# A gated recurrence and a squared-ReLU MLP on one core: other order of the first loads, three opening pairs by halves, second weights rounded one group ahead, a reordered last group

## What is computed

```python
# x, f_logit: (2, 6080, 256); lower_bound: (256,)
f = lower_bound + (1 - lower_bound) * sigmoid(f_logit)
h = f[:, t] * h + (1 - f[:, t]) * x[:, t]        # for t in range(6080), y[:, t] = h
# the MLP over all 12160 tokens; w_in: (256, 2048), w_out: (2048, 256)
hidden = y.reshape(12160, 256) @ w_in
g = maximum(hidden, 0) ** 2
out = g @ w_out
```

## Time and profile before

| | |
|---|---|
| median of 3 runs | 992.76 us (992.21 to 994.01) |
| the profiled execution | 992.73 us, of which its span is 990.7 us |
| PE busy | 985.3 us (99%), 4394 matmuls |
| PE weight loads busy | 819.2 us (83%) |
| DVE busy | 731.2 us (74%) |
| ACT busy | 697.3 us (70%) |
| POOL busy | 48.3 us (5%) |
| PE clock granted | full in all 40 slices |
| DMA | 8 tenths busy in the first slice (24.8 us), 309 GB/s; 42 GB/s over the span |
| the chain that ended last | PE 99%, DVE 1% |

### The profile page before, as it was taken

How to read it: one execution, slowest core, us unless ns; L and a number is a source line. 1 busy time by engine, 2 the same in 40 slices (tenths; PEclk the granted TensorE clock), 3 DMA queues, 4 the chain that set the end, 5 groups by cost and what they waited for, 6 DMA issues and landing times.

```text
span 990.7 us, 12612 instructions
## 1 busy us (share of the span) xinstructions
PE 985.3 (99%) x4394; PEld 819.2 (83%) x4394; DVE 731.2 (74%) x939; ACT 697.3 (70%) x924; POOL 48.3 (5%) x50
## 2 busy tenths in 40 slices
PE   9999999999999999999999999999999999999998
PEld 7898888888888888888888888888888888888887
DVE  6897876887787688687687768768768777876545
ACT  7876766776776776676677677677667767766665
POOL 2673000000000000000000000000000000000000
PEclk9999999999999999999999999999999999999999
DMA  8003011102101201100210110110111021001001
GB/s 309 21 1 109 14 43 43 43 1 85 43 1 43 85 0 42 64 21 0 85 42 0 55 72 0 42 64 21 34 51 42 0 85 43 1 0 43 1 1 43
DMA packets 22159, 41.95 MB, mean 42 GB/s; under 512 B 1521, under 2 KB 3313, under 8 KB 22129
## 3 DMA queue, kind: packets, MB, share of 16 engines
q1 hardware_dynamic: 21984, 41.43, 12.1%
q10 hardware_dynamic: 144, 0.13, 0.0%
HBM read 29.10 MB, written 12.45 MB: 42 GB/s over the span
## 4 chain that ended last, share of the span: by engine, by line
PE 99%; DVE 1%; issue 0%; ACT 0%; POOL 0%; DVEq 0%; ACTq 0%; POOLq 0%
PE out_ps L849 52%; PE hidden_ps L835 42%; PE hidden_ps L875 3%; PE out_ps L869 1%; PE out_ps L875 1%; PE out_ps L859 1%; DVE x_in L512 0%; DVE w_out_lo L613 0%; ACT g_hi L361 0%; POOL zeros L811 0%; DVE result L771 0%; DVE result L776 0%; DVE result L773 0%; DVE g_lo L625 0%; DVEq L775 0%
## 5 line engine op out<-in xcount | busy, mean ns | idle before, releaser
L849 PE MATMUL out_ps<-g_hi,w_out_hi 128*128 128x512 f32 (+1 forms) x760 | 294.3, 387 | 1.2 <-DVE w_out_lo L613 1.2
L849 PE MATMUL out_ps<-g_lo,w_out_hi 128*128 128x512 f32 (+1 forms) x760 | 294.1, 387 | 0.0
L849 PE MATMUL out_ps<-g_hi,w_out_lo 128*128 128x512 f32 (+1 forms) x760 | 294.1, 387 | 0.0
L625 DVE TENSOR_TENSOR g_lo<-h,g_hi 128x1024 fp32r<-128x1024 f32 (+1 forms) x190 | 232.6, 1224 | 69.8 <-ACT g_hi L361 66.8
L354 ACT ACTIVATE h<-h 128x1024 f32<-128x1024 f32 (+1 forms) x190 | 200.2, 1054 | 3.2
L849 PEld LDWEIGHTS out_ps<-g_hi,w_out_hi 128*128 128x128 f32 x760 | 142.6, 188 | 29.9 <-DVE w_out_lo L613 1.6
L849 PEld LDWEIGHTS out_ps<-g_lo,w_out_hi 128*128 128x128 f32 x760 | 142.7, 188 | 28.3
L849 PEld LDWEIGHTS out_ps<-g_hi,w_out_lo 128*128 128x128 f32 x760 | 142.6, 188 | 28.1
L835 PE MATMUL hidden_ps<-sums_hi,wc_hi 128*128 128x512 f32 x352 | 137.1, 389 | 0.0
L835 PE MATMUL hidden_ps<-sums_lo,wc_hi 128*128 128x512 f32 x352 | 137.0, 389 | 0.0
L835 PE MATMUL hidden_ps<-sums_hi,wc_lo 128*128 128x512 f32 x352 | 136.9, 389 | 0.0
(11 more groups left out here) (109 smaller groups left out, 1050.1 us busy)
## 6 DMA issues: line engine op xcount, KB each, us to landing
x_in<-x_t SPq DMA_DIRECT2D x22, 512.0 KB, 4.4
f_in<-f_logit_t SPq DMA_DIRECT2D x22, 512.0 KB, 4.7
out_t<-result SPq DMA_DIRECT2D x20, 512.0 KB, 3.1
w_in_raw<-w_in_t SPq DMA_DIRECT2D x8, 256.0 KB, 6.3
w_out_raw<-w_out_t SPq DMA_DIRECT2D x8, 256.0 KB, 7.3
x_in<-x_first SPq DMA_DIRECT2D x4, 224.0 KB, 5.4
out_t<-result SPq DMA_DIRECT2D x2, 448.0 KB, 3.0
out_t<-result SPq DMA_DIRECT2D x3, 256.0 KB, 2.0
```

Of the source, the lines that this page charges most:

```text
L625: nc.vector.tensor_tensor(g_lo[b][:, :, 0:n], h_of(it, j, b), g_hi[b][:, :, 0:n].bitcast(F32), ALU.subtract).then_inc(g_ready[b], 1)
L849: mm = nc.tensor.matmul(out_ps[:, b, c, 0:n], half[:, j, m, c * P:(c + 1) * P], moving[b][:, m, 0:n], start=(j == 0 and m == 0 and k == 0) ...
```

## The change

- The constants: 16 in place of 20 zero matmuls at the start, 2 in place of 4 between the halves.
- Loads: the second half's f is issued ahead of `w_in` 0, and `w_in` 2 ahead of batch 1's pieces.
- ACT: the second half's gate comes ahead of the rounding of `w_in` 0; `w_in` 2 is rounded right behind `w_in` 1, ahead of batch 1's gate and of `half_y_hi(1)`.
- DVE: `half_y_lo(0)` comes behind the second half's scans; `half_y_lo(1)` ahead of the rest of `w_in` 1.
- PE: three pairs of batch 0 instead of two are done by halves in their hi-by-hi pass; all passes with the lo values come in full width behind both halves.
- `w_out` 2 to 6 are each rounded, and their rests formed, one group earlier, `w_out` 1 earlier within the first group; `w_out` 7 stays where it is.
- The last group of the last tile has its own order, `last_quad`: the passes of the previous group's products are split among `product7`, `product4` and `product3`.

```diff
-WARM_UP = 20
-FILL = 4
+WARM_UP = 16
+FILL = 2
...
         def w_out_quads(j):
-            return (j, j + 1) if j == QUADS - 2 else (j,) if j < QUADS - 2 else ()
+            return (j + 1,) if j < QUADS - 1 else ()
...
             load_first_f(0, 0)
             load_first_x(0, 0)
+            load_first_f(0, 1)
             load_w_in(0)
-            load_first_f(0, 1)
             load_first_x(0, 1)
             load_w_in(1)
+            load_w_in(2)
             load_first_f(1, 0)
             load_first_x(1, 0)
             load_first_f(1, 1)
             load_first_x(1, 1)
-            load_w_in(2)
             load_w_out(0)
...
                 plain_w_in_hi(3)
                 first_relu(2, 0)
+                round_w_out(1)
                 first_relu(0, 1)
...
                 square_pair(0, 1, 1)
-                round_w_out(1)
+                round_w_out(2)
                 gate(1, 0, 0)
...
+            gate(0, 0, 1)
             plain_w_in_hi(0)
-            gate(0, 0, 1)
             for c in range(C):
                 half_forget(1, c)
             plain_w_in_hi(1)
+            plain_w_in_hi(2)
             gate(0, 1, 0)
             half_y_hi(1)
             first_forget(1, 0)
             gate(0, 1, 1)
             first_forget(1, 1)
-            plain_w_in_hi(2)
             first_y_hi(1, 0)
...
                     lo_pair(0, 0, 0)
+                    rest_of_w_out(1)
                     lo_pair(0, 0, 1)
                     lo_pair(0, 1, 0)
-                    rest_of_w_out(1)
+                    rest_of_w_out(2)
...
             first_w_in_lo(0)
-            half_y_lo(0)
             for c in range(C):
                 half_input(1, c)
                 half_scan(1, c)
+            for k in range(2):
+                half_y_lo(k)
             first_w_in_lo(1)
-            half_y_lo(1)
...
-            def first_two_pairs0():
+            def first_three_pairs0():
 
                 for k in range(2):
                     pe.wait_ge(first_hi_done[0][k], 1)
-                    for j in range(2):
+                    for j in range(3):
                         pe.wait_ge(w_plain_hi_done, j + 1)
                         for c in range(C):
 
                             first_part(j, 0, c, wc_hi, hi_of, opens=k == 0 and c == 0, columns=part(k))
-                        if j == 0:
+                        if (k, j) == (0, 0):
                             rests_of_w_in(0)
                             for c in range(C):
-                                first_part(0, 0, c, wc_lo, hi_of, columns=part(k))
-                        if k == 0:
-                            pe.wait_ge(first_ready[0][0], 1)
-                            for c in range(C):
-                                first_part(j, 0, c, wc_hi, lo_of, columns=part(0))
+                                first_part(0, 0, c, wc_lo, hi_of, columns=part(0))
                     if k == 0:
                         warm(FILL)
-                rests_of_w_in(1)
                 for c in range(C):
-                    first_part(1, 0, c, wc_lo, hi_of)
-                pe.wait_ge(first_ready[0][1], 1)
-                for j in range(2):
-                    first_part(j, 0, 0, wc_hi, lo_of, columns=part(1))
-                    first_part(j, 0, 1, wc_hi, lo_of, columns=part(1), signal=pair_done[0])
+                    first_part(0, 0, c, wc_lo, hi_of, columns=part(1))
+                for k in range(2):
+                    pe.wait_ge(first_ready[0][k], 1)
+                for j in range(3):
+                    first_part(j, 0, 0, wc_hi, lo_of)
+                    if j == 0:
+                        first_part(0, 0, 1, wc_hi, lo_of, signal=pair_done[0])
+                    else:
+                        first_part(j, 0, 1, wc_hi, lo_of)
+                        rests_of_w_in(j)
+                        first_part(j, 0, 0, wc_lo, hi_of)
+                        first_part(j, 0, 1, wc_lo, hi_of, signal=pair_done[0])
...
                 product5(it, odd, j)
+                if very_last(it, j):
+                    last_quad(it, odd, j, prev)
+                    return
...
+            def last_quad(it, odd, j, prev):
+
+                second(*prev, 0, 0, 1, passes=(0,))
+                product7(it, odd, j)
+                second(*prev, 0, 0, 1, passes=(1, 2))
+                second(*prev, 0, 1, 0, passes=(0, 1))
+                product4(it, odd, j)
+                second(*prev, 0, 1, 0, passes=(2,))
+                second(*prev, 0, 1, 1, passes=(0, 1))
+                product3(it, odd, j)
+                second(*prev, 0, 1, 1, passes=(2,))
+                second(*prev, 1, 0, 0)
```

More of the change, by code:

```diff
@@ L837, in product, with second @@
                 mm.then_inc(signal, 1)
-            def second(it, j, b, m, c):
+            def second(it, j, b, m, c, passes=range(3)):
                 n, q = width(it), it * QUADS + j
-                if m == 0 and c == 0:
+                if m == 0 and c == 0 and 0 in passes:
                     if narrow(it) and b == 0:
@@ L847, in second @@
                     pe.wait_ge(g_ready[b], q + 1)
-                for k, (half, moving) in enumerate(((w_out_hi, g_hi), (w_out_hi, g_lo), (w_out_lo, g_hi))):
+                for k in passes:
+                    half, moving = ((w_out_hi, g_hi), (w_out_hi, g_lo), (w_out_lo, g_hi))[k]
                     mm = nc.tensor.matmul(out_ps[:, b, c, 0:n], half[:, j, m, c * P:(c + 1) * P],
@@ L851, in second @@
                                           stop=False, skip_group_check=True)
-                if m == 1 and c == 1:
+                if m == 1 and c == 1 and 2 in passes:
                     mm.then_inc(g_used[b], 1)
@@ L965, in first_quad @@
                 if j == 0:
-                    first_two_pairs0()
-                    first_pair0(2)
+                    first_three_pairs0()
                     first_two_pairs1()
@@ L1032, in quad @@
                 second(*prev, 0, 1, 0)
-                if not very_last(it, j):
-                    second(*prev, 0, 1, 1)
+                second(*prev, 0, 1, 1)
                 product4(it, odd, j)
[L1036 to L1039, removed]
+                second(*prev, 1, 0, 0)
                 product3(it, odd, j)
-                if very_last(it, j):
-                    second(*prev, 1, 0, 0)
+                second(*prev, 1, 0, 1)
+                second(*prev, 1, 1, 0)
+                second(*prev, 1, 1, 1)
+            def last_quad(it, odd, j, prev):
[8 more added lines that the diff above has]
+                second(*prev, 0, 1, 1, passes=(2,))
+                second(*prev, 1, 0, 0)
                 second(*prev, 1, 0, 1)
```

## The result

The changed kernel takes 990.88 us (median of 22 runs, 990.22 to 991.84) against 992.70 (22 runs, 992.21 to 994.01): ratio 0.9982, 95% interval 0.9975 to 0.9988. That is 1.82 us less, where 1.62 was forecast, inside the range. The profiled execution is one of the slower ones: 991.41 us, span 989.4, so the two traces are only 1.32 apart. The other 0.5 us of the gain shows in the medians and not in these two executions.

The account below looks back on a forecast made before the run. TensorE (PE), busy 985.3 of 990.7 us, was taken as the bound. From the profiled 992.73, 0.24 + 0.03 lost and 1.48 + 0.41 gained gave -1.62, so 991.1; range 990.2 to 992.4, own range 990.6 to 991.6.

Parts of the forecast that it names:

- What bounds the kernel: Whole kernel: PE is busy for 985.3 of 990.7 us, so an edit counts only if it moves PE.
- The stall, 1.48: PE's wait for `w_out_lo` near 37 us goes when the second weights are rounded one group earlier: 1.48 us gained.
- What is late next: After the stall, `second(2,0)` and `second(3,0)`: VectorE is near full from 36 to 56 us, but no use comes nearer than 1.2 us.
- The last group, 0.41: Last group of the last tile: the new order puts the last products in place at 981.73, 0.41 us gained, bounds 0.15 to 0.5.
- DMA order: Opening loads: `w_in` 0 lands at 7.02 instead of 6.25, `w_in` 2 at 9.35, f of batch 1 at 10.06.
- Rivals A and B: Start: A, it gains a little, 990.7, chance 0.18; B, it loses more through late loads, 991.7, chance 0.15.
- Pairs' end, 17.25: Start: the three opening pairs on PE end at 17.25 instead of 17.01, 0.24 us lost.
- Warm-ups and fills worth nothing: Start: dropping four warm-ups (0.86 us) and two fills (0.43) gains nothing, as PE's idle takes them.
- ACT's chain to `first_relu(1, 1)`: Behind the start: later relus and the added `round_w_out(1)`, 0.6 us, cost 0.03 us, range 0 to 0.4.
- Rival C, the clock: Start: the engine's clock returns to 1.2 GHz or rises late; 993.9 for a low stretch of 5.5 us; chance 0.06.
- The sum, 1.62 against 1.82: Whole kernel: 0.24 + 0.03 - 1.48 - 0.41 = -1.62 us was forecast, so 991.1.
- the start's 0.27: Start: the predicted loss, 0.24 us at the opening pairs' end and 0.03 in ACT's chain behind it.

Follow-up runs that it names:

- x1: The kernel before with only the second weights' rounding and rests moved one group earlier: 991.19 us against 992.68, ratio 0.9983.
- x2: The kernel before with only the last group's own order, `last_quad`: 992.28 us, ratio 0.9995.
- x3: The kernel before with only the new start (loads, ACT and DVE order, three pairs by halves, 16 and 2 zero matmuls): 992.97 us, ratio 1.0001.
- z1: The changed kernel again, unchanged, for a second profile of its start: 991.05 us, ratio 0.9982 to the kernel before.
- y1: The changed kernel with 20 and 4 zero matmuls again in place of 16 and 2: 990.87 us, ratio 0.9984 to the kernel before.
- y4: The changed kernel with the second half's scans freed from `w_in` 0, `half_forget` and `half_y_hi(1)` ahead on ACT: 990.45 us, ratio 0.9977 to the kernel before.
- x4: The changed kernel with the old start put back (second weights and last group as changed): 990.98 us, ratio 0.9982 to the kernel before.
- y2: The changed kernel with `w_in` 0 again ahead of the second half's f, in loads and on ACT: 990.94 us, ratio 0.9981 to the kernel before.
- y3: x4 with 16 and 2 zero matmuls in the old start: 990.47 us, ratio 0.9979 to the kernel before.
- z2: y4 with no zero matmuls between the halves (`FILL = 0`): 990.71 us, ratio 0.9980 to the kernel before.
- w2: y4 with `first_relu(1, 1)` ahead of `hi_pair(0, 1, 0)` on ACT: 990.65 us, ratio 0.9978 to the kernel before.
- w1: x4 with `first_relu(1, 1)` ahead of `hi_pair(0, 1, 0)` on ACT, removing PE's wait at 27 us: 991.68 us, ratio 0.9989 to the kernel before.

## Why the prediction was right, and where it was not

- **What bounds the kernel**: right. Every gain is one in PE's sequence, and what was hidden stayed hidden.
- **The stall, 1.48**: right in place and size (x1: 1.49). What I had not seen is its second price: behind each restart the first tile's matmuls can run at the higher pitch, 0.95 us behind the one at 38, in a minority of executions. In the mean instead of the median x1 gains 1.60 (992.86 to 991.26). How often the unprofiled executions took the higher pitch is read from their times alone.
- **What is late next**: right, nothing. `second(3, 0)` has no wait in any trace without the stall.
- **The last group, 0.41**: 0.40 by the traces, 0.40 by x2's medians (the interval includes 0). The size is right partly by luck. The forecast left 0.17 us of loss in this stretch, 0.13 of it by `product4` (two restarts and 0.04 of slower pitch) and the rest at the last products. 0.18 is left (10.38 against 45 pitches, 10.20), but made otherwise: `product7` cost 0.04 and `product4` 0.01; `g_lo` (to 980.66) still released the last weight load, yet the products began at 980.80 with 0.02 of extra duration. The largest part, 0.1, is in the 15 matmuls from 974.34, which start 0.233 us apart instead of 0.2267.
- **DMA order**: 7.02 for the landing of `w_in` 0 was a fair middle and a bad number. By issue and time to landing it came at 6.32 to 7.52 in the seven profiles with the new order (7.52 in the changed kernel's) and at 6.05 to 6.65 in the seven with `w_in` 0 first. The order costs 0.5 in the mean, the execution as much as 1.2. Rivals A and B, meant as alternatives, are both seen as executions of the same kernel.
- **Pairs' end, 17.25**: 17.55, 17.09 and 16.50 in three executions, and 16.74 in x3. The one whose cast was where I had put it (z1, 7.05) ended 0.16 from the forecast. The half that failed is the other side: I took the 10.47 of one profile for the second half's cast in the old start, which begins there between 10.41 and 10.89 in the six profiles of it, and in the new start between 9.93 and 10.91. The pairs' end is 16.97 in the mean of the four profiles with the new start and 16.99 in the six with the old one, so over executions no loss of 0.24 shows. That `half_y_hi(1)` would be held by the landing of batch 1's f came true in y1 only, where ACT waited 0.22 us for that f at 9.41. In the changed kernel's profile and in z1 DVE's scan released it (0.33 of idle on ACT), because the residual of `w_in` 0 stood ahead of the scans, and y4, which turns that around, moved it to 9.32.
- **Warm-ups and fills worth nothing**: right (y1: 990.87 against 990.88). The moment at which the clock rises from 1.2 to 2.4 GHz varies between executions, with the same unbroken row of zeros ahead of it: their pitch halved at 6.85 in the kernel before and at 4.71 in x1:

```profile
4.28 0.15 PEld L871 LDWEIGHTS out_ps<-zeros 128*128 128x128 bf16 x1 [0.28 <-issue]
4.71 2.32 PEld L871 LDWEIGHTS out_ps<-zeros 128*128 128x128 bf16 x11 [0.28 <-issue]
```

- **ACT's chain to `first_relu(1, 1)`**: 0.03 was forecast, and in this trace it is nothing (the restart moved from 26.93 to 27.47, just as the pairs' end did), so `round_w_out(1)` cost nothing. But I had costed this restart at its 0.1 us of waiting, and it is the point at which the pitch of the following 56 us is drawn.
- **Rival C, the clock**: did not occur. PE paused for some 2 us in the changed kernel's start (from 7.3 to 11.53 it does 16 x 0.1125 + 2 x 0.216 = 2.2 us of work; 1.6 was forecast), and the pitch of the 224-column matmuls stayed at 0.11. The Trainium skill ("TensorE: Matmul & The Clock Gate", Part 1) says that the slow clock is the default and activity releases it. I had set this against the change, and it did not bite at these pauses, of which the longest is 0.8 us.
- **The sum, 1.62 against 1.82**: the term that was mis-sized is the start's 0.27. In its place the traces show no loss in the mean, and the medians show 0.29 (x3) and -0.12 (the changed kernel's 1.82 against x4's 1.70), each within 0.9. That the missing loss makes up the difference of 0.20 is likely and not shown, since a sum within 0.2 is closer than these runs can tell.

Open: what decides the pitch at a restart. The restarts at 27 in the kernel before, x1, x2, x4, y2, y3 and the changed kernel's first profile all led from 0.2067 to 0.2025, that of z1 did not, and those of x2 and x3 at 38 led to 0.2067. The other profiles (x3, y1, y4, z2, w2) opened at 0.2025 already. In all 14 the opening's pitch goes with ACT's cast of the second half: 0.2025 in these five, where it began between 9.32 and 10.18, and 0.2067 in the nine where it began at 10.41 or later. No run tests whether the one causes the other. Open too is why the start that frees the scans has two groups of times.

## What to carry to other kernels

Read a landing time from several executions before building an order on it: the landing of one load varied by 1.2 us between executions, more than the reorder cost (0.5). Sum terms where one engine is the bound: the removed stall (1.48 forecast, 1.47 by the traces) and the reordered last group (0.41 and 0.40) came out in size, even where the restarts inside the second did not. And when the engine that bounds the kernel is at 99%, compare the pitch of equal matmuls between stretches and executions, not only its waits.

## What the hardware showed that I had not expected

Float32 matmuls of 448 columns with their weight loads run in one of two steady pitches, 0.2025 or 0.2067 us, which held for up to some 270 matmuls and changed in these 14 profiles only where PE had to wait and restarted; the wait that seems to cost 0.1 us can be worth 0.7 us of time in the other direction (w1). The same code, loads and data gave both. The time from issue to landing of one 256 KB load at the start of the kernel was 4.4, 4.9 and 5.4 us in three executions of the same load order.
